# 304 more matmuls behind the last product of a token mix followed by two feed-forward stages

## What is computed

```python
def _attn_ref(x, weight):                      # x (2, 4096, 192), weight (8, 7)
    w = softmax of weight over its 7 taps
    x_pad = np.concatenate([zeros(B, 6, D), x], axis=1)
    out = np.einsum('hk,bskhg->bshg', w, x_unf)   # causal mix of 7 tokens, one set of taps per head
    return out

def _moe_ref(x, w_gate, w_val, w_out):         # (8192, 192), w_gate and w_val (192, 1536), w_out (1536, 192)
    g = x @ w_gate
    silu = g * (1.0 / (1.0 + np.exp(-g)))
    return silu * (x @ w_val) @ w_out

def _moe2_ref(x, w_in, w_out):                 # w_in (192, 2048), w_out (2048, 192)
    h = x @ w_in
    g = np.where(h > 0.0, h, np.exp(np.minimum(h, 0.0)) - 1.0)
    return g @ w_out
```

## Time and profile before

| | value |
|---|---|
| median of 2 runs | 1180.19 us |
| the profiled execution: its time | 1180.13 us |
| its span, first to last instruction | 1178.3 us |
| PE busy | 1173.2 us, 100% of the span, 11802 matmuls |
| PEld busy | 1168.7 us |
| DVE, ACT, POOL busy | 758.0, 666.9, 697.9 us |
| chain that ended last | PE 100% |

### The profile page before, as it was taken

One profiled execution on the slowest core, in us unless ns is written; L12 is line 12 of the kernel. 1 busy time (PEld: TensorE's weight loads), 2 busy tenths in 40 slices (PEclk: granted clock), 3 DMA queues, 4 the chain that ended last, 5 costly groups with the idle time before them and its releaser, 6 DMA issues.

```text
span 1178.3 us, 31406 instructions
## 1 busy us (share of the span) xinstructions
PE 1173.2 (100%) x11802; PEld 1168.7 (99%) x11802; DVE 758.0 (64%) x1193; ACT 666.9 (57%) x1115; POOL 697.9 (59%) x517
## 2 busy tenths in 40 slices
PE   9999999999999999999999999999999999999999
PEld 8999999999999999999999999999999999999998
DVE  7878565675646666566664756647567475675665
ACT  6557555464654646556465564655646556465565
POOL 6378565474654746547465474655757456475565
PEclk9999999999999999999999999999999999999999
DMA  7512011121101211012110021200212002120110
GB/s 175 126 42 46 19 29 33 32 45 31 25 19 31 45 31 28 17 31 45 31 36 18 22 45 31 44 9 22 45 31 45 9 22 45 31 45 9 33 33 15
DMA packets 103444, 43.24 MB, mean 37 GB/s; under 512 B 75376, under 2 KB 93424, under 8 KB 103408
## 3 DMA queue, kind: packets, MB, share of 16 engines
q1 hardware_dynamic: 102848, 42.36, 16.1%
q10 hardware_dynamic: 560, 0.39, 0.1%
HBM read 15.99 MB, written 6.29 MB: 19 GB/s over the span
## 4 chain that ended last, share of the span: by engine, by line
PE 100%; ACT 0%; issue 0%; DVE 0%; ACTq 0%
PE up L907 56%; PE down L907 44%; PE down L1111 0%; ACT hidden L648 0%; ACT in_a_hi L655 0%; DVE stage L746 0%; ACT stage L675 0%; DVE halos L831 0%; ACTq L644 0%
## 5 line engine op out<-in xcount | busy, mean ns | idle before, releaser
L452 POOL TENSOR_TENSOR hid_lo<-hidden,hid_hi 128x512 fp32r<-128x512 f32 x435 | 598.3, 1389 | 454.8 <-ACT hid_hi L591 295.7
L907 PE MATMUL down<-out_w,hid_hi 64*128 64x384 f32 x2040 | 303.4, 353 | 0.0
L907 PE MATMUL down<-out_w,hid_lo 64*128 64x192 f32 x2040 | 292.5, 247 | 0.0
L768 DVE TENSOR_TENSOR hidden<-act,up 128x512 f32<-128x512 f32 x191 | 131.0, 686 | 234.8 <-ACT act L574 234.7
L907 PE MATMUL up<-in_b_hi,up_w_hi 64*128 64x512 f32 x1128 | 246.7, 388 | 0.0
L809 DVE TENSOR_SCALAR act<-up 128x512 f32<-128x512 f32 x256 | 164.7, 685 | 126.0 <-PE up L907 124.3
L907 PE MATMUL up<-in_b_hi,up_w_lo 64*128 64x512 f32 x1128 | 245.8, 387 | 0.0
L907 PE MATMUL up<-in_b_lo,up_w_hi 64*128 64x512 f32 x1128 | 245.7, 386 | 0.0
L907 PEld LDWEIGHTS down<-out_w,hid_lo 64*128 64x128 f32 x2040 | 242.2, 187 | 0.0
L907 PEld LDWEIGHTS down<-out_w,hid_hi 64*128 64x128 f32 x2040 | 238.9, 184 | 0.2 <-issue 0.2
L591 ACT ACTIVATE hid_hi<-hidden 128x512 fp32r<-128x512 f32 x192 | 121.5, 633 | 176.6 <-DVE hidden L768 159.0
(11 more groups left out here) (100 smaller groups left out, 1201.9 us busy)
## 6 DMA issues: line engine op xcount, KB each, us to landing
x_raw<-x_dram SPq DMA_DIRECT2D x136, 64.0 KB, 2.2
out_dram<-stage SPq DMA_DIRECT2D x15, 384.0 KB, 2.7
in_b_hi<-in_b_hi SPq DMA_DIRECT2D x32, 128.0 KB, 2.3
in_b_lo<-in_b_lo SPq DMA_DIRECT2D x32, 128.0 KB, 2.3
swapped<-halves SPq DMA_DIRECT2D x32, 128.0 KB, 2.3
in_a_hi<-in_a_hi SPq DMA_DIRECT2D x30, 128.0 KB, 2.3
in_a_lo<-in_a_lo SPq DMA_DIRECT2D x30, 128.0 KB, 2.3
stage<-w_out_dram SPq DMA_DIRECT2D x7, 384.0 KB, 4.0
```

What stands on the lines that cost most here:

```text
L452: return pool.tensor_tensor(hid_lo[:, slot, :], hidden[:, s, :], hid_hi[:, slot, :].bitcast(F32), ALU.subtract)
L768: v.tensor_tensor(hidden[:, f % 2, :], act[:, f % 2, :], val_bank(f, n)[:, :], ALU.mult)\
L907: return nc.tensor.matmul(dst, lhsT, rhs, start=start, stop=stop, skip_group_check=True)
```

## The change

A function `spare_time` is added to PE's program and called once, behind `last_blocks`. It holds 304 matmuls, with no wait and no signal, that read tiles whose contents are no longer needed (`in_a`, `out2_w`, `up1_w`) and write the four `up` banks, which nothing reads any more. No other engine's program changes. The seven pieces of the function, which I call A to G:

| piece | in each round | rounds | matmuls |
|---|---|---|---|
| A | wide top, wide low, narrow top, narrow low | 12 | 48 |
| B | wide top, narrow low, wide low, narrow top, in the same two banks | 12 | 48 |
| C | as B, the narrow ones in two other banks | 12 | 48 |
| D | as A, the narrow ones with 96 instead of 128 columns loaded | 12 | 48 |
| E | narrow top, narrow low, then two of 512 streamed columns with 66 loaded | 12 | 48 |
| F | 512 streamed columns top and low, 128 loaded | 8 | 16 |
| G | 12 wide pairs, then 12 narrow pairs | 24 pairs | 48 |

```diff
+            def spare_time():
+                flat = {k: in_a[k][:, :, :].rearrange("p s t -> p (s t)") for k in ("hi", "lo")}
+                banks = {TOP: up[1], LOW: up[2]}
+                spare = {TOP: up[0], LOW: up[3]}
+
+                def tokens(part, rows, i, held=P, into=banks):
+                    cols = slice(0, 2 * D if part == "hi" else D)
+                    mm(into[rows][0:held, cols], flat[part][rows, 0:held], out2_w[rows, i % 8, cols], True, True)
+
+                def channels(i, rows, wpart, part, width=P, into=banks):
+                    mm(into[rows][0:width, :], up1_w[wpart][rows, MAIN, i % 8 * P:i % 8 * P + width],
+                       flat[part][rows, 0:T], True, True)
+
+                for i in range(12):
+                    for part in ("hi", "lo"):
+                        for rows in (TOP, LOW):
+                            tokens(part, rows, i)
+                for i in range(12):
+                    tokens("hi", TOP, i)
+                    tokens("lo", LOW, i)
+                    tokens("hi", LOW, i)
+                    tokens("lo", TOP, i)
+                for i in range(12):
+                    tokens("hi", TOP, i)
+                    tokens("lo", LOW, i, into=spare)
+                    tokens("hi", LOW, i)
+                    tokens("lo", TOP, i, into=spare)
+                for i in range(12):
+                    for rows in (TOP, LOW):
+                        tokens("hi", rows, i)
+                    for rows in (TOP, LOW):
+                        tokens("lo", rows, i, 96)
+                for i in range(12):
+                    for rows in (TOP, LOW):
+                        tokens("lo", rows, i)
+                    for rows in (TOP, LOW):
+                        channels(i, rows, "hi", "lo", 66, spare)
+                for i in range(8):
+                    channels(i, TOP, "hi", "hi")
+                    channels(i, LOW, "lo", "hi", into=spare)
+                for part in ("hi", "lo"):
+                    for i in range(12):
+                        for rows in (TOP, LOW):
+                            tokens(part, rows, i)
+
@@
             elu_phase(CHUNKS)
             last_blocks()
+            spare_time()
```

## The result

The changed kernel takes 1200.57 us (median of 2 runs, 1200.57 to 1200.58) against 1180.19: a ratio of 1.0173, 95% interval 1.0156 to 1.0189. That is 20.4 us more; 20.2 were forecast, and the range was 1199.1 to 1202.8.

The account below looks back on a forecast made before the run. PE was taken to bound the kernel. From its last matmul at 1175.13, 0.20 for the shape change, the priced pieces A to G and 0.25 for the meeting end the span at 1198.5; plus 1.83 gives 1200.35 us, range 1199.1 to 1202.8.

Parts of the forecast that it names:

- The cover: Behind PE's last real matmul, a 2.9 us gap until the span ends hides added matmuls; what is longer sets the end.
- The change of rows: Ahead of A, the tile shape goes from 128 to 64 rows: +0.20 us, bounds 0 and 0.4.
- A step is the longer of stream and load: Between added pairs, a step is the longer of streaming this one and loading the next: 0.284 us per wide-narrow round.
- Independent halves: In B and C each row half needs 0.284 us a round whatever its partner does, so they cost as much as A.
- rival 1: In B and C, a matmul must not end before the one ahead: rounds of 0.342, +1.4 us, 1201.7; chance 0.20.
- rival 2: In B and C, out of step is cheaper, wide loads hidden: rounds of 0.259, -0.6 us, 1199.75; chance 0.06.
- rival 3: In B and C, unlike matmuls don't run beside each other: rounds of 2 x 0.284, 1207.2 us; chance 0.04.
- Rival 4: Narrow loads of D and E change the tile shape, about 0.20 each: 48 changes, +9.6 us, 1210; chance 0.03.
- Rival 5: The clock falls: all of the added part at 1.2 GHz adds another 23 us, 1223; chance 0.02.
- the meeting of the engines: After the last narrow pair ends, the engines meet before the span ends: 0.25 us, bounds 0.1 and 0.44.

Follow-up runs that it names:

- the run with 8 rounds: Changed kernel with only 8 rounds of piece A, pieces B to G left out: 1180.14 us against 1180.24 for the kernel before, ratio 0.9999.
- the shape run: Changed kernel with A to G replaced by pieces alternating 128 with 64 rows, then 128 with 64 loaded columns: 1222.25 us.
- the run with wide pairs between: Changed kernel with A to G replaced by pairs of 64 streamed columns, loading 32, 64, 66, 96, 128, each piece followed by 24 wide pairs: 1207.0 us.
- The run with 64 streamed columns: Changed kernel with A to G replaced by six pieces of 24 pairs streaming 64 columns, loading 128, 96, 66, 64, 32, 128: 1192.91 us.

## Why the prediction was right, step by step

- **The cover.** Right: the run with 8 rounds costs nothing, and the overhang sets the end in the full one.
- **The change of rows.** 0.20 taken, 0.18 in the trace of the changed kernel, 0.20 on average over 55 changes of the shape run.
- **A step is the longer of stream and load.** Right. A, B, C: 0.284 for the top half's round. D 0.287 (taken 0.284, +0.03 us in all). E 0.320 (the top half's 12 rounds reach from 1189.20 to 1193.04 in the trace), taken 0.315: +0.06, and the load of 66 columns is hidden, as taken. F 0.230 for the top half ((1194.87 - 1193.04)/8; 0.227 taken, +0.02). G 0.176 for a wide step (0.171 taken, +0.06), 0.112 for a narrow one, but the first narrow step is 0.088, since its load lies behind a wide stream (-0.03). The price of the load itself, which I had only read from two record lengths, is 0.109 us for 128 columns and 0.060 for 66 by the run with wide pairs between.
- **Independent halves.** The conclusion was right and the picture behind it wrong. I had argued that the starts fall in the program's order anyway (0, 0.05, 0.16, 0.17 in a round), so that nothing had to be passed. The low half in fact drifted further back than that, and the order is left: in the last round of C a narrow matmul of the top half starts at 1185.67, ahead of the low half's wide one (1185.72) that stands before it in the program. The experiments show how deep the halves overtake each other: three matmuls. That a kept order would have made the lag cost time in the narrow pairs of G (0.14 against steps of 0.11) is only argued. That the low half lags 0.05 in the earlier trace rows was no evidence for it; in A of the changed kernel the lag is under 0.01.
- **Rivals 1, 2 and 3**: rounds of 0.285 in B and C leave no room for 0.34, 0.26 or 0.57. For rival 1 (0.20) the 48 narrow starts beside 45 wide ones come on top; I had said that the trace of before has no pair to tell, and that holds. **Rival 4**: 0.008 at most for a change of columns. **Rival 5**: the steps stayed those of the upper level to the end. The run with 64 streamed columns shows that a fall of the clock was a rival to be taken seriously: there it came with PE busy throughout.
- **The rest.** The last real product starts at 1175.26 in this execution, 0.13 later than in the profiled one of before, the low half's lag adds 0.14 (0.05 of it was in the sum, as part of the 0.30 of a joined pair), and the meeting of the engines takes 0.24 (0.25 taken). The span comes out 0.3 over the forecast, the median 0.2: small errors that partly cancel. The range is a little wider than its own terms give: 1199.75 - 0.5 is 1199.25, not 1199.1, and 1201.7 + 1.0 is 1202.7, not 1202.8. The result lies well inside either.

No run points to a version that beats the kernel before: the added matmuls are pure cost beyond the gap, and the real rounds already stand at the longer of stream and load. What could be gained there is the 0.03 by which a load of 128 columns outlasts a stream of 192 (0.113 against some 0.085, which is my estimate from 0.227 for 512), and it needs other operand shapes. This wasn't tried.

## What to carry to other kernels

Price matmuls by the distance of their starts, as the longer of their own stream and the next load in the same half of the rows (here 0.109 us for 128 loaded columns and 0.79 ns less for each column fewer), and each half by itself. For matmuls of 368 or 384 streamed columns the order between two halves is free in blocks of four, and blocks of eight cost 14%; a half gets ahead of the other's place in the program by three matmuls and no more. Gather work over 64 rows and over 128 rows, since each change between them costs 0.2 us here, and use the time of the last stores for nothing longer than they are.

## What the runs showed of the hardware that I had not expected

- The two row halves pass each other in their starts: with three matmuls of one half still waiting, one that stands behind them in the program starts on the other.
- A PE that is busy without a gap can lose its clock: with loads of 128, 96 and 66 columns, each followed by only 64 streamed ones from 1175.3 on, the granted clock fell to 0.50 at 1181.1. With pieces of wide pairs between, the steps stayed those of the upper level.
- Two halves in the same program order can settle at a round of 0.284 or, one of them, at 0.290. What decides is open.
